# Expert stage of a fused attention and mixture-of-experts kernel: routing work moved between layers, weight pieces reordered

## The chip, the cores and the metric

The kernel runs on 1 core of one Trainium2 chip. The metric is the device time of one execution in microseconds (us). TensorE is called PE in the profile, VectorE is DVE, ScalarE is ACT, GpSimd is POOL, SyncE is SP (here it only starts DMAs). Each engine works through its own queue in order and meets the others at semaphores.

## What is computed

Three steps in a row. A recurrent attention (4 batches, 8 heads, 768 steps, width 40) gives 3072 rows of 320 numbers. A mixture of 8 experts then takes these rows, where each expert must get exactly 384 of them:

```python
logits = x @ w_gate
order = np.argsort(-logits.flatten())
for idx in order:                       # best (row, expert) pairs first
    tok, e = idx // E, idx % E
    if assigned[tok] >= 0 or counts[e] >= cap: continue
    assigned[tok] = e; counts[e] += 1
for e in range(E):
    h = np.maximum(x[assigned == e] @ w1[e], 0.0)
    out[assigned == e] = h @ w2[e]
```

The last step is one more network on every row, `g = elu(x @ w_in); y = g @ w_out`, of width 2048.

## The kernel before

**Stages.** The attention runs to about 206 us of the span and is not touched. `experts` then handles one expert after the other, in the order in which they fill up. For expert k it does a first layer pair (`up`, `down`: 320 to 1024 to 320) and, on the same 384 rows, the last network (`up2`, `down2`: 320 to 2048 to 320, called the second layer here). The hidden width is cut in slices of 128: 8 slices u in the first layer (`NF`), 16 slices f in the second (`NF2`). Every product is made of high and low parts: 8 matmuls of 384 columns for a slice of `up`, `down` or `up2`, 9 matmuls of 320 columns for a slice of `down2`.

**A second-layer slice on four engines.** PE makes `up2(f)` into one of three PSUM banks (`ring`). ACT makes negation, tanh and exp of it (`elu` on ACT), DVE combines them in two instructions (L1274, L1277), ACT rounds the result to its high part `gl_hi` (L1405), POOL subtracts to get the low part `gl_lo` (L1024), and PE multiplies both in `down2(f)`, three slices behind (`LAG`). `up2(f)` for f of 3 or more waits until DVE has finished slice f - 3, whose bank it writes into: `pe.wait_ge(g_ok, k * NF2 + f - 2)`.

**Routing.** The rows of expert k + 1 are found while expert k is computed. DVE and PE alternate in 7 rounds (`ROUNDS`): DVE compares all scores with up to 31 thresholds (`round_compare`, L1112), PE counts the takers with 24 small matmuls (`count_takers`, L1463), DVE tests (`round_test`), PE counts the thresholds passed with one matmul (`count_thresholds`, L1469), DVE moves the base (`round_move`). Then follow `choose_counts`, `totals` (PE), `choose_expert` (which also releases the weight fetch of that expert on SP), `prefix` (PE), `choose_ties`, `prefix` again, `choose_leave`, `choose_spots` (24 DVE instructions, L1233, that fill a one-hot table), `list_tokens` (24 matmuls, L1484) and `choose_tokens`, which gives the row numbers. POOL's `gather` fetches the rows with three indirect DMAs (L1003) and `columns` transposes them (PE L1495, ACT, DVE).

**Where it stands before.** Rounds 1 to 7 for the expert after next run in the second layer of expert k, one in every two slices; the rest of that routing in the first layer of expert k + 1. `choose_spots` stands in two halves at slices 6 and 7 of the first layer, its table shares memory with the buffers of the second layer (`unit`). Expert 0 has no expert ahead of it: its routing runs alone, and so do five rounds of expert 1.

**Weights.** SP fetches pieces into two staging buffers, ACT rounds the high part (`split_hi`), POOL subtracts for the low part (`split_lo`), and only then is the buffer free for the piece after next. The output weights `w_out` (8 pieces) come first, during the routing of expert 0. An expert's own 8 pieces (4 of `w1`, then 4 of `w2`) are worked on in the second layer of the expert before, one at every even slice.

## Time and profile before

| | us |
|---|---|
| median of 3 runs (lowest, highest) | 885.33 (883.17, 887.6) |
| the profiled execution | 887.74 |
| its span, first to last instruction | 886.0 |
| PE busy in the span | 790.1 |
| DVE, ACT, POOL busy | 527.8, 461.4, 421.1 |

The span is what the trace shows; 1.7 us lie around it. A busy PE is a PE with a matmul in its pipeline, so gaps count for more than the share. The span has three parts: attention to about 206 us, a stretch in which PE is mostly idle to about 264 us, and then eight experts, one about every 77 us.

### The profile page before, as it was taken

To read this page: it belongs to the slowest core of one execution; us is meant where nothing else is said; L and a number is where in the kernel's file an instruction comes from. 1 tells how busy PE (TensorE), PEld (TensorE's weight loads), DVE (VectorE), ACT (ScalarE), POOL (GpSimd) and SP (SyncE) were. 2 spreads that over 40 slices of the span, in tenths; PEclk is the share of its full clock that TensorE was granted. 3 is DMA by queue.
4 is the path that set the end of the run, shared out by engine and by line. 5 is a ranking of instruction groups with operands and counts; after the bars stand their busy time and mean duration, and the time that the engine had idled before them with its cause. 6 is when DMAs were issued, how large, how long until landed. Compare 5 with 4: busy or idle time off the path is not lost.

```text
span 886.0 us, 19502 instructions
## 1 busy us (share of the span) xinstructions
PE 790.1 (89%) x6470; PEld 734.4 (83%) x6470; DVE 527.8 (60%) x1535; ACT 461.4 (52%) x981; POOL 421.1 (48%) x467
## 2 busy tenths in 40 slices
PE   1999999994249999999999999999999999999994
PEld 1788888883139899989989989998999899899894
DVE  7475666666774864765476476547647655543441
ACT  1444444431231676387277538726763872784573
POOL 6444444443360475085257508525750852474133
PEclk9999999996557999999999999999999999999998
DMA  3978787842241120121212012121201211120000
GB/s 65 143 135 137 130 135 129 138 79 89 88 124 42 45 67 23 58 80 46 65 46 66 31 53 80 43 68 44 67 24 58 80 46 65 46 79 24 0 2 22
DMA packets 138521, 61.12 MB, mean 69 GB/s; under 512 B 104704, under 2 KB 136704, under 8 KB 138432
## 3 DMA queue, kind: packets, MB, share of 16 engines
q1 hardware_dynamic: 136128, 52.13, 27.1%
q0 software_dynamic: 2304, 7.87, 2.8%
q8 instruction: 48, 0.79, 0.4%
q14 instruction: 41, 0.34, 0.1%
HBM read 51.72 MB, written 8.26 MB: 68 GB/s over the span
## 4 chain that ended last, share of the span: by engine, by line
PE 54%; DVE 7%; POOL 5%; issue 4%; ACT 4%; DMA 1%; SPq 1%; ACTq 0%; POOLq 0%; DVEq 0%
PE bank L1503 6%; PE bank L1573 6%; PE bank L1504 5%; PE bank L1507 5%; PE bank L1574 5%; PE bank L1575 5%; PE bank L1463 3%; PE bank L1511 3%; PE bank L1509 3%; PE bank L1547 3%; PE bank L1549 3%; PE bank L1548 3%; DVE cmp L1112 2%; POOL gl_lo L1024 1%; PE bank L1532 1%
## 5 line engine op out<-in xcount | busy, mean ns | idle before, releaser
L1024 POOL TENSOR_TENSOR gl_lo<-unit,gl_hi 128x384 fp32r<-128x384 f32 x128 | 133.8, 1045 | 128.0 <-ACT gl_hi L1405 127.4
L1573 PE MATMUL bank<-Wo_hi,gl_hi 128*128 128x320 f32 x384 | 123.7, 322 | 5.0 <-POOL gl_lo L1024 5.0
L1574 PE MATMUL bank<-Wo_lo,gl_hi 128*128 128x320 f32 x384 | 118.7, 309 | 0.0
L1575 PE MATMUL bank<-Wo_hi,gl_lo 128*128 128x320 f32 x384 | 118.7, 309 | 0.0
L1274 DVE SCALAR_TENSOR_TENSOR unit<-bank,unit 128x384 f32<-128x384 f32 x104 | 57.8, 556 | 94.2 <-ACT bank L1398 93.9
L1373 ACT ACTIVATE hid_hi<-bank 128x384 fp32r<-128x384 f32 x64 | 31.4, 491 | 133.7 <-PE bank L1511 133.7
L1003 POOL DMA_INDIRECT xg<-x_rows,idx x24 | 23.7, 989 | 157.9 <-PE bank L1511 90.4
L1503 PE MATMUL bank<-x_hi,Wi_hi 128*128 128x384 f32 x256 | 92.3, 360 | 2.0 <-DVE unit L1277 0.9
L1390 ACT ACTIVATE unit<-bank 128x384 f32<-128x384 f32 x128 | 62.0, 484 | 51.3 <-PE bank L1511 50.2
L1504 PE MATMUL bank<-x_hi,Wi_lo 128*128 128x384 f32 x256 | 86.2, 337 | 0.0
L1573 PEld LDWEIGHTS bank<-Wo_hi,gl_hi 128*128 128x128 f32 x384 | 72.2, 188 | 6.8 <-POOL gl_lo L1024 6.7
L1277 DVE TENSOR_TENSOR unit<-unit,bank 128x384 f32<-128x384 f32 x128 | 70.9, 554 | 4.4
L1574 PEld LDWEIGHTS bank<-Wo_lo,gl_hi 128*128 128x128 f32 x384 | 72.2, 188 | 0.0
L1575 PEld LDWEIGHTS bank<-Wo_hi,gl_lo 128*128 128x128 f32 x384 | 72.1, 188 | 0.0
L1393 ACT ACTIVATE unit<-unit 128x384 f32<-128x384 f32 x128 | 67.3, 525 | 4.4
L1463 PEld LDWEIGHTS bank<-pick,cmp 128*128 128x128 bf16 x1344 | 38.4, 99 | 36.0 <-DVE cmp L1112 24.7
L1405 ACT CAST gl_hi<-unit 128x384 fp32r<-128x384 f32 x128 | 63.8, 499 | 6.3 <-DVE unit L1277 6.2
L1463 PE MATMUL bank<-pick,cmp 128*128 128x8 bf16 x1344 | 43.3, 167 | 25.6 <-DVE cmp L1112 25.3
L1257 DVE SCALAR_TENSOR_TENSOR hid_lo<-bank,hid_hi 128x384 fp32r<-128x384 f32 x64 | 35.4, 554 | 51.4 <-ACT hid_hi L1373 50.8
L1507 PE MATMUL bank<-x_lo,Wi_hi 128*128 128x384 f32 x256 | 65.9, 339 | 0.0
L316 POOL TENSOR_SCALAR_AFFINE_SELECT W<-W 128x512 f32<-128x512 f32 x48 | 35.4, 761 | 61.2 <-ACT W L490 61.2
L442 DVE TENSOR_TENSOR PW<-bank,W 128x512 f32<-128x512 f32 x48 | 30.9, 686 | 50.2 <-PE bank L551 45.6
(244 smaller groups left out, 2122.8 us busy)
## 6 DMA issues: line engine op xcount, KB each, us to landing
stage<-in_moe_w_dram SPq DMA_DIRECT2D x32, 320.0 KB, 2.9
stage<-in_moe_w_dram SPq DMA_DIRECT2D x32, 256.0 KB, 2.6
stage<-in_moe_w_dram SPq DMA_DIRECT2D x96, 64.0 KB, 2.4
q_in<-in_q_dram SPq DMA_DIRECT2D x24, 160.0 KB, 3.2
k_in<-in_k_dram SPq DMA_DIRECT2D x24, 160.0 KB, 3.9
o_in<-in_o_gate_dram SPq DMA_DIRECT2D x24, 160.0 KB, 4.1
v_in<-in_v_dram SPq DMA_DIRECT2D x24, 160.0 KB, 4.1
x_rows<-xt SPq DMA_DIRECT2D x24, 160.0 KB, 1.9
```

The costliest lines, as they stand in the source:

```text
L1024: nc.gpsimd.tensor_tensor(gl_lo[:, b, :], ex[:, b, :], gl_hi[:, b, :].bitcast(F32), ALU.subtract).then_inc(gl_ok, 1)
L1277: nc.vector.tensor_tensor(ex[:, b, :], ex[:, b, :], ring[(NF + f) % 3][:, 0:CAP], ALU.max).then_inc(g_ok, 1)
L1390: nc.scalar.activation(ex[:, b, :], ring[(NF + f) % 3][:, 0:CAP], ACT.Relu, scale=-1.0).then_inc(neg_ok, 1)
L1393: nc.scalar.activation(th[:, f % 2, :], ex[:, b, :], ACT.Tanh, scale=-0.5).then_inc(th_ok, 1)
L1405: nc.scalar.copy(gl_hi[:, b, :], ex[:, b, :]).then_inc(gl_hi_ok, 1)
L1463: ins = nc.tensor.matmul(pR[:, 0:E], cmp_w[:, g * NT:g * NT + P], pick[:, g, :], start=(g == 0), stop=(g == G - 1))
L1503: nc.tensor.matmul(to, w_hi[:, c, cols], x_hi[m][:, c, :], start=(c == 0), stop=False)
L1504: nc.tensor.matmul(to, w_lo[:, c, cols], x_hi[m][:, c, :], start=False, stop=False)
L1507: nc.tensor.matmul(to, w_hi[:, c, cols], x_lo[m][:, c, :], start=False, stop=False)
L1573: nc.tensor.matmul(acc[j][:, 0:DM], gl_hi[:, f % RG, t_], Wo_hi[:, f, :], start=(f == 0), stop=False)
L1574: nc.tensor.matmul(acc[j][:, 0:DM], gl_hi[:, f % RG, t_], Wo_lo[:, f, :], start=False, stop=False)
L1575: ins = nc.tensor.matmul(acc[j][:, 0:DM], gl_lo[:, f % RG, t_], Wo_hi[:, f, :], start=False, stop=(f == NF2 - 1))
```

## The change

- Of the 7 rounds for the next expert only rounds 1 and 2 stay in the second layer of the expert before (slices 11 to 15). Rounds 3 to 7 stand at slices u = 2 to 6 of the first layer, `choose_counts` to `choose_ties` at its end.
- `choose_leave` and both halves of `choose_spots` stand on DVE between the two layers, ahead of slice 0 of the second; `spot` has a buffer of its own. `list_tokens` stands on PE behind `up2(3)`, `choose_tokens` on DVE ahead of slice 3, `gather` on POOL behind slice 1. `TURN`, the slice of the first transposes, goes from 12 to 9.
- The high part `gl_hi` of even slices is made by DVE instead of ACT.
- Pieces of an expert come in the order of `PIECES`; five of them are worked on in the second layer of the expert before (slices 0, 4, 6, 8, 10), three in the expert's own first layer (u = 2, 3, 4).
- `w_out` is fetched behind the pieces of expert 0: three pieces are worked on in the first layer of expert 0 (u = 5, 6, 7), five in its second (slices 0, 1, 3, 4, 5). Ahead of expert 0 POOL has the gather first, then five pieces.
- Ahead of the first matmul only rounds 1 and 2 of expert 1 remain, and the three transposes stand together.

```diff
-    spot = unit[:, 0:G * P // 2].bitcast(FP16).rearrange("p (g c) -> p g c", g=G)
+    spot = sb("spot", [P, G, P], FP16)
...
+    PIECES = ((True, 0), (True, 1), (False, 0), (True, 2), (False, 1), (True, 3), (False, 2), (False, 3))
+    EARLY = 5
...
+    def in_up(k, u):
+        own = [(None, EARLY + u - 2)] if u - 2 < PER - EARLY else []
+        late = [(u - 5, None)] if isinstance(k, int) and k == 0 and u >= 5 else []
+        return own + late
+    def in_up2(k, f, after):
+        if isinstance(k, int) and k == 0:
+            outs, at = (0, 1, 3, 4, 5), (7, 9, 11, 13, 15)
+        else:
+            outs, at = (), (0, 4, 6, 8, 10)
...
-    TURN = NF2 - NJ - 1
+    TURN = 9
...
@@ gpsimd
-                gather(k + 1, 1 - s)
             for f in range(NF2):
                 elu_lo(k, f)
-                if f % 2 == 0 and after:
-                    expert_rest(k + 1, f // 2)
+                for i, at in in_up2(k, f, after):
+                    w_out_rest(i) if at is None else expert_rest(k + 1, at)
+                if f == 1 and after:
+                    gather(k + 1, 1 - s)
...
@@ vector
             for u in range(2, NF):
+                q = u + 1
+                if after and q <= ROUNDS:
+                    round_compare(c, q)
+                elif after:
+                    choose_counts(c)
+                hidden(k, u - 1)
+                if after and q <= ROUNDS:
+                    round_test(c, q)
+                    round_move(c, q)
+            if after:
+                choose_expert(c)
+            hidden(k, NF - 1)
+            if after:
+                choose_ties(c)
             between_layers(k)
             if after:
-                choose_tokens(c, 1 - s, n + s)
+                choose_leave(c)
+                for part in range(SPOTS):
+                    choose_spots(c, part)
             for f in range(NF2):
+                if f == 3 and after:
+                    choose_tokens(c, 1 - s, n + s)
...
@@ tensor
                 up(k, u)
+                if after and q <= ROUNDS:
+                    count_takers(c, q)
...
                 down(k, u - 2)
+                if after and q <= ROUNDS:
+                    count_thresholds(c, q)
...
                 if f < NF2:
                     up2(k, f)
+                if f == 3 and after:
+                    list_tokens(c)
```

How the rows stand in the queues. First DVE, from the end of the first layer of expert 0 to its first second-layer slice; `x_lo1` is the input of the second layer, `hid_lo` a slice of the first. Before:

```order
L1233 TENSOR_SCALAR unit<-slots,row 128x128 x12
L1257 SCALAR_TENSOR_TENSOR hid_lo<-bank3,hid_hi 128x384
L1233 TENSOR_SCALAR unit<-slots,row 128x128 x12
L1257 SCALAR_TENSOR_TENSOR hid_lo<-bank4,hid_hi 128x384
...
L1268 TENSOR_TENSOR x_lo1<-unit,x_hi1 64x384
...
L1274 SCALAR_TENSOR_TENSOR unit<-bank6,unit 128x384
L1277 TENSOR_TENSOR unit<-unit,bank5 128x384
```

And after the change:

```order
L1301 TENSOR_TENSOR x_lo1<-unit,x_hi1 64x384
L1233 SCALAR_TENSOR_TENSOR L<-taken,L 128x192
...
L1256 SCALAR_TENSOR_TENSOR L<-sel,L 128x192
L1266 TENSOR_SCALAR spot<-slots,row 128x128 x24
L1307 SCALAR_TENSOR_TENSOR unit<-bank6,unit 128x384
L1310 TENSOR_TENSOR unit<-unit,bank5 128x384
L1314 CAST gl_hi<-unit 128x384
L1307 SCALAR_TENSOR_TENSOR unit<-bank6,unit 128x384
```

The 24 instructions of `choose_spots`, and the 10 of `choose_leave` ahead of them, moved from among the slices of the first layer to a place between `x_lo1` and the first slice of the second layer.

Then POOL, from the start of the second layer of expert 1. Before:

```order
L1003 DMA xg<-x_rows,idx0 128x320 x3
L1024 TENSOR_TENSOR gl_lo<-unit,gl_hi 128x384
L764 TENSOR_TENSOR W1_lo<-stage0,W1_hi 128x2x256
L767 TENSOR_TENSOR W1_hi<-stage0,W1_hi 128x256
L1024 TENSOR_TENSOR gl_lo<-unit,gl_hi 128x384 x2
```

And after the change:

```order
L1056 TENSOR_TENSOR gl_lo<-unit,gl_hi 128x384
L764 TENSOR_TENSOR W1_lo<-stage0,W1_hi 128x2x256
L767 TENSOR_TENSOR W1_hi<-stage0,W1_hi 128x256
L1056 TENSOR_TENSOR gl_lo<-unit,gl_hi 128x384
L1028 DMA xg<-x_rows,idx0 128x320 x3
L1056 TENSOR_TENSOR gl_lo<-unit,gl_hi 128x384 x3
```

The gather moved from ahead of `gl_lo` of slice 0 to between those of slices 1 and 2.

Last PE, from the transposes of expert 0's rows to its first products. Before:

```order
L1495 MATMUL bank6<-ident,xg 64x128
L1463 MATMUL bank7<-pick,cmp 128x8 x24
L1469 MATMUL bank7<-feas,first31 128x1
L1495 MATMUL bank6<-ident,xg 128x128 x2
L1495 MATMUL bank6<-ident,xg 64x128
L1463 MATMUL bank7<-pick,cmp 128x8 x24
L1469 MATMUL bank7<-feas,first15 128x1
L1503 MATMUL bank3<-x_hi0,W1_hi 128x384
```

And after the change:

```order
L1537 MATMUL bank6<-ident,xg 64x128
L1537 MATMUL bank6<-ident,xg 128x128 x2
L1537 MATMUL bank6<-ident,xg 64x128
L1505 MATMUL bank7<-pick,cmp 128x8 x24
L1545 MATMUL bank3<-x_hi0,W1_hi 128x384
```

The counts that stood between and behind the transposes are gone from here, but for one.

## Rows read from the trace of the kernel before

**Rows 1.** page, part 1: busy us (share of span) xinstructions, by engine
```profile
PE 790.1 (89%) x6470; PEld 734.4 (83%) x6470; DVE 527.8 (60%) x1535; ACT 461.4 (52%) x981; POOL 421.1 (48%) x467
```

**Rows 2.** windows: busy us per engine in each, PE clock, DMA share, GB/s
```profile
206.00:232.00 26.00, 8.38 (x181) 7.00 (x181) 14.83 (x43) 5.80 (x8) 13.79 (x11) 0.50 0.35 103
...
272.00:277.00 5.00, 4.56 (x17) 4.42 (x16) 2.47 (x12) 0.49 (x1) 0.00 (x0) 0.50 0.00 2
...
277.00:282.00 5.00, 5.00 (x33) 4.84 (x32) 1.83 (x11) 0.49 (x1) 0.00 (x0) 0.99 0.00 0
...
380.00:460.00 80.00, 78.88 (x633) 74.07 (x634) 49.83 (x156) 49.85 (x109) 42.38 (x42) 1.00 0.18 54
```

**Rows 3.** timeline, first routing: start us, us, engine, line, out<-in, [idle before]
```profile
213.59 1.53 POOL L770 TENSOR_TENSOR Wo_lo<-stage,Wo_hi 128x640 fp32r<-128x640 f32 x1
...
213.73 2.19 DVE L1112 SCALAR_TENSOR_TENSOR cmp<-hi,base,ramps 128x744 bf16<-128x744 f32 x1
...
238.00 6.66 DVE L1233 TENSOR_SCALAR unit<-slots,row 128x128 f16<-128x128 f16 x24
...
240.73 1.30 POOL L764 TENSOR_TENSOR W_lo<-stage,W_hi 128x512 fp32r<-128x512 f32 x1 [8.55 <-ACT W_hi L755]
```

**Rows 4.** line L1112, one form: ns min/median/max, first to last start
```profile
L1112 DVE SCALAR_TENSOR_TENSOR cmp<-hi,base,ramps x16: 1024/1039/2235, 213.7 to 700.1; 128x744 bf16<-128x744 f32 x16
```

**Rows 5.** timeline, from routing of expert 1 to second layer of expert 0
```profile
246.02 0.34 DVE L1071 TENSOR_REDUCE best<-L 128x24 f32<-128x192 f32 x1
...
254.36 0.88 PE L1495 MATMUL bank<-ident,xg 128*128 128x128 f32 x3
...
261.58 0.87 PE L1495 MATMUL bank<-ident,xg 128*128 128x128 f32 x3
...
264.46 0.66 PE L1503 MATMUL bank<-x_hi,W_hi 128*128 128x384 f32 x1
...
295.72 0.42 PE L1503 MATMUL bank<-x_hi,Wi_hi 128*128 128x384 f32 x1
```

**Rows 6.** timeline, PE, threshold count 3 and taker count 4, expert 0
```profile
221.17 0.19 PE L1469 MATMUL bank<-feas,first 128*128 128x1 bf16 x1 [0.43 <-DVE feas L1122]
...
223.07 0.81 PE L1463 MATMUL bank<-pick,cmp 128*128 128x8 bf16 x24 [1.71 <-DVE cmp L1112]
```

**Rows 7.** timeline, DVE, around the start of a steady second layer
```profile
439.27 0.21 DVE L1206 TENSOR_TENSOR_SCAN incl<-bank,zeros 128x24 f32<-128x24 f32 x1 [2.02 <-PE bank L1479]
...
441.15 0.56 DVE L1257 SCALAR_TENSOR_TENSOR hid_lo<-bank,hid_hi 128x384 fp32r<-128x384 f32 x1
...
444.04 2.03 DVE L1233 TENSOR_SCALAR unit<-slots,row 128x128 f16<-128x128 f16 x12
...
450.05 0.55 DVE L1268 TENSOR_TENSOR x_lo<-unit,x_hi 64x384 fp32r<-64x384 f32 x1 [0.51 <-ACT x_hi L1383]
...
452.91 0.56 DVE L1274 SCALAR_TENSOR_TENSOR unit<-bank,unit 128x384 f32<-128x384 f32 x1 [0.52 <-ACT bank L1398]
...
453.50 0.56 DVE L1277 TENSOR_TENSOR unit<-unit,bank 128x384 f32<-128x384 f32 x1
```

**Rows 8.** timeline, PE, the same second layer
```profile
454.11 0.45 PE L1503 MATMUL bank<-x_hi,Wi_hi 128*128 128x384 f32 x1 [0.24 <-DVE unit L1277]
...
455.62 0.76 PE L1463 MATMUL bank<-pick,cmp 128*128 128x8 bf16 x24
...
463.24 0.39 PE L1573 MATMUL bank<-Wo_hi,gl_hi 128*128 128x320 f32 x1
```

**Rows 9.** timeline, POOL, the same second layer
```profile
454.65 1.07 POOL L1003 DMA_INDIRECT xg<-x_rows,idx  x1 [0.31 <-issue]
...
456.76 1.31 POOL L764 TENSOR_TENSOR W_lo<-stage,W_hi 128x512 fp32r<-128x512 f32 x1
...
458.01 0.76 POOL L767 TENSOR_TENSOR W_hi<-stage,W_hi 128x256 fp32r<-128x256 f32 x1
```

**Rows 10.** waits of PE after 277 us: total us, times, longest us
```profile
PE bank L1463 <- DVE cmp L1112: 2.1, 3, 1.0
```


## What I predict, and why

> **What bounds the kernel now.** I read the busy shares first, then the windows by stage, then the timeline of three places. PE is busy for 790 of 886 us [rows 1]: the kernel is bound by PE wherever PE can work. The windows show where it can't. From 206 to about 264 us it has a matmul in flight for a small part of the time (8.4 of the first 26 us) and runs at a granted clock of 0.5, the level of 1.2 GHz; in the middle of the expert stage it is busy for 78.9 of 80 us at 1.00, 2.4 GHz [rows 2]. So there are two prices. A microsecond cut from the serial stretch before the first expert is a microsecond gained. In the steady part nothing can be gained beyond some 1 us of waiting for each expert (78.9 of 80), and any new wait of PE is paid in full, seven times, since seven of the eight experts carry the routing of a next one.
>
> **The start: a gain of about 9 us.** Ahead of expert 0 the change takes all work from POOL and ACT that does not belong to the routing. What is it worth? DVE's comparison with `base` takes 2.19 us beside POOL's subtraction, which began 0.14 us before it [rows 3]; the median of this form is 1.04 us [rows 4]. Two such comparisons run in the first routing: 2 x 1.15 = 2.3 us. The 24 instructions of `choose_spots` took 6.66 us there, beside POOL's splits of `w1` [rows 3], and 2.03 us for 12 in the steady part, where POOL is idle [rows 7]: 6.66 - 4.06 = 2.6 us. With 0.3 us for the last comparison the routing of expert 0 ends 5.2 us earlier, and that of expert 1 begins at 240.8 instead of 246.0 [rows 5].
>
> From there to the first product before: 264.46 - 246.02 = 18.4 us [rows 5]. After: the first transposes have one round less ahead of them. A round is a comparison of 1.04, a count of 0.81 and three small steps, about 3 us in all (0.19 + 1.71 us from threshold count to taker count are the shorter part of one [rows 6]). So they start 254.36 - 246.02 - 3.0 = 5.3 us behind the routing's begin, at 246.1. The row of the last transposes is followed by the first product 2.9 us later [rows 5]; without counts between, all three sets should keep this pitch (before they took 3.6): 246.1 + 3 x 2.9 = 254.8. That is 9.7 us earlier. The weights are ready: POOL does its gather from about 242 to 245.5 and needs 1.31 + 0.76 us for a `w1` piece [rows 9].
>
> From the first product to the second layer of expert 0 it took 295.72 - 264.46 = 31.3 us. Five rounds are added in there (count and restart about 0.9 each, 4.4 in all, and some 1.3 of waits, below); two rounds with PE waiting through most of them (about 1.3 each), the 24 matmuls of `list_tokens` (0.6) and part of the stretch at 1.2 GHz go (about 2). I take +0.5, so the second layer of expert 0 starts **9.2 us earlier**. Bounds of this term: 6 if weight pieces, which now come three to the first layer, hold `up` or `down` once; 12 if the clock rises early.
>
> **The second layer: a new wait of about 4 us, then one of 2.** This is the term that decides. Before, DVE finishes `x_lo` at 450.05 + 0.55 = 450.6, has 2 us of small routing work, and takes slice 0 at 452.91, when ACT's exp is ready [rows 7]. PE has by then done three slices into the three banks of `ring`; its fourth starts at 454.11, just behind DVE's second instruction, after an idle 0.24 us [rows 7, 8]. So DVE's slice 0 is already what PE meets first.
>
> The change puts `choose_leave` and all of `choose_spots` ahead of that slice, in the same queue. `choose_leave`: 441.15 - 439.27 = 1.9 us for the part behind the prefix and 0.3 for two instructions ahead of it; `choose_spots`: 2 x 2.0 us [rows 7]. Together 6.2 us, from 450.6 to 456.8. Slice 0 then ends at 456.8 + 1.15 = 457.95 instead of 454.06, and `up2(3)` starts at **457.9, not 454.1: 3.8 us later**, behind 4 us of an idle PE. Nothing can fill them: PE's next instruction is this one, and its data are in no other engine's hands.
>
> Then POOL. Before, the gather is issued while nothing else wants POOL; its last issue starts at 454.65 and `gl_lo` of slice 0 follows. Now it stands behind slice 1, and behind a piece of `w1`. DVE's new cast of `gl_hi` has no row; it reads and writes 384 columns in SBUF. Its bounds are 0.2 (12 one-source instructions of 128 columns take 2.03, 0.17 each) and 0.56, what the two-operand instructions of 384 columns take [rows 7]; I take 0.35, nearer to the one-source rows. Then: 457.95 + 0.35 = 458.3; `gl_lo(0)` to 459.35 (1.0 us, the distance of slice 0's to the next row of POOL); the piece, 1.31 + 0.76 with a little overlap, to 461.4 [rows 9]; `gl_lo(1)` to 462.4; the gather, three issues of about 1.27, to 466.4; `gl_lo(2)` to 467.5. PE needs it for `down2(2)`. Counted from 457.9, it has `up2(3)`, `up2(4)`, `up2(5)` at 1.4 (454.11 to 455.62 is 1.5 with a restart [rows 8]), `list_tokens` 0.6 and two `down2` of 1.4, and gets there at 465.5. So it waits 2.1 us more, to about 467.7. Before, `down2(2)` started at 463.24 [rows 8]. PE is 4.45 us later, and has one count (0.8 with its restart) less behind it: 5.25 us of new waiting. The waits of the comparisons that leave this layer were 2.1 us in all after 277 us [rows 10], 0.35 for each expert. **Net 4.9 us for each of 7 experts, 34.3 us.** For expert 0 POOL has a second piece of `w_out` ahead of the gather (1.57 instead of nothing, less 0.5 for the smaller first one): +1.1.
>
> DVE's cast takes from ACT 0.5 us every second slice. ACT was no bound (49.9 of 80 us [rows 2]), so this gives nothing; DVE (49.8) has room for it.
>
> The row of 2.19 us bears on that cast: DVE stood still until POOL was through [rows 3]. The Trainium skill (SBUF — State Buffer, section Terms) has the rule: VectorE and GpSimd share one pair of ports, exclusively for a whole instruction, and the loser is blocked. By it the cast of slice 2 would wait out the piece of `w1` and hold POOL for itself, 0.4 us more before `gl_lo(2)`, 2.8 us over seven experts; without it nothing. The sum is made with half of that, inside the 467.7.
>
> **The first layer.** Rounds 3 to 7 now stand between `up` and `down`. PE's work for them is the same as in the second layer. Their chain runs from the threshold count through DVE's move and comparison to the next taker count, and has only one `up` of 1.4 us to hide in. For round 4, with its two more instructions, it is 223.07 - 221.17 = 1.9 us [rows 6]: a wait of 0.5. Rounds 5 to 7 have half as many thresholds and fit, but two of them meet a weight piece on POOL and can be held by up to its 1.31 us [rows 9]; I take 0.3 each. The first taker count covers 0.2 us that `down(0)` waited before. Net 0.9 us, for six experts 5.4 (expert 0's are in the term above). Bounds: 0 and 3 us for each expert.
>
> **The sum**, against the profiled execution: 887.7 - 9.2 + 34.3 + 1.1 + 5.4 = 919.3. The median of the runs is 2.4 us below that execution: **917 us**, 3.6% slower.
>
> **Rivals.**
> (1) The clock falls in the new wait of 4 us. Where PE was idle for stretches of a microsecond and more, it ran at 0.50, and came back to 1.00 only after it had worked without a gap from about 272.5 to 277 [rows 2]. In the 5 us before it did 17 matmuls, in the 5 us behind 33: such a stretch loses 2.5 us. A part is absorbed by the wait for POOL behind it; with a second fall there I take 2 us net for an expert: 917 + 14 = 931, up to 938 with 3 us. Against it: idle of half a microsecond never lowered it in the steady part [rows 2], and for 4 us there is no row. The Trainium skill (TensorE: Matmul & The Clock Gate, section Why this matters for your kernels) warns that idle gaps between bursts of matmuls bring the lower clock back; by it the time would be this rival's 931, by the rows it is open.
> (2) POOL keeps up: the first piece or the gather costs PE no second wait. Then 2.2 us less for each expert, 917 - 15 = 902. For it: POOL's times are rough; against it: three issues in a row stand in its queue.
> (3) Faster than before: the start decides. This needs less than 9.2 / 7 = 1.3 us of new waiting for each expert, so DVE would have to be through with `choose_leave` and `choose_spots` in about 3.5 us, not 6.2, because exp(0) came later or the 24 instructions ran faster from their own buffer. With no such wait the time is 885.3 - 9.2 + 5.4 - 2.5 = 879. Against it: the fastest rows for 12 of them are 2.03 us.
>
> **How the numbers follow.** My forecast with its own range (908 to 926) has 0.52, rival 1 0.20, rival 2 0.14, rival 3 0.08, something between before and 900 that I don't see 0.06. The range reaches to rivals 1 and 2 and leaves out rival 3 and the ends: 899 to 938. Beyond 0.5% (4.4 us, about what a measurement of this kernel can tell from no change): faster 0.08, within 0.03, slower 0.89.
>
> **What would show it.** In the changed profile: the first product at about 255 us; the comparisons of the first routing at 1.0 us; 24 `spot` instructions in 4 us right before DVE's slice 0, and PE idle about 4 us before the fourth slice of each second layer, put down to DVE; then about 2 us put down to POOL's `gl_lo`; a second-layer period of 81 to 83 us for each expert instead of 77. I am wrong if PE's longest waits there are under 1.5 us, or if the clock row shows levels under 1.00 in the steady part.

## The result, and the profile after

The changed kernel takes **942.2 us** (939.6 to 942.6, four runs) where the kernel before takes 886.5 on the same chip (883.2 to 892.0, four runs): a ratio of **1.062**, 95% interval 1.056 to 1.067. The forecast was 917 us with a range of 899 to 938. The direction, the start and the main wait came as forecast. The size didn't: 25 us of loss were missed, more than the range allowed.

The page of the changed kernel, part 1, as [rows 1]:

```profile
PE 806.9 (86%) x6470; PEld 745.6 (79%) x6470; DVE 593.1 (63%) x1599; ACT 436.1 (46%) x917; POOL 422.5 (45%) x467
```

PE has the same 6470 instructions, is busy 17 us longer for them (790.1 before) and idle 37 us longer (133 against 96 us). The longer work for the same matmuls goes with the lower clock: the mean granted clock is 0.941 over 940.1 us, where it was 0.955 over 886.0, so 55 us of full clock are missing instead of 40. The windows say where (us, then busy us of PE, PEld, DVE, ACT, POOL, then PE clock, DMA share, GB/s): one of 80 us as in [rows 2], one inside the new wait, and one behind each of two waits.

```profile
380.00:460.00 80.00, 72.94 (x582) 68.02 (x581) 53.01 (x134) 43.18 (x92) 39.63 (x38) 0.96 0.18 53
...
386.50:390.30 3.80, 0.03 (x1) 0.00 (x0) 3.77 (x20) 1.16 (x4) 0.00 (x0) 1.00 0.00 0
...
391.40:394.60 3.20, 3.20 (x35) 2.96 (x34) 2.95 (x9) 2.34 (x5) 3.20 (x4) 0.56 0.00 0
447.00:449.80 2.80, 2.80 (x10) 2.49 (x10) 0.40 (x3) 0.00 (x0) 1.38 (x2) 0.50 0.41 117
```

In 80 us PE is busy for 72.9 where it was for 78.9. It is idle from 386.5 to 390.3 at full clock, works on, and about 1.4 us later the clock goes to 0.50, its level of 1.2 GHz. The same happens again behind a shorter wait at 446 us.

Waits of PE behind 277 us, as [rows 10] (total us, times, longest us). Before, the longest in the steady part were about 1 us.

```profile
PE bank L1545 <- DVE unit L1310: 27.0, 7, 3.9
PE bank L1505 <- DVE cmp L1145: 10.6, 6, 2.1
PE bank L1537 <- DVE unit L1307: 6.3, 6, 3.5
PE bank L1617 <- POOL gl_lo L1056: 4.9, 8, 2.1
```

The first line is the fourth slice of each second layer, the second the comparison of round 4 in the first layer (2.0 to 2.1 us in five experts, 0.4 in the sixth), the third the transposes of the next tokens, the fourth `down2`. Together they are 49 us; the loss is 56. Here is the first of them in the timeline (start us, us, engine, line, out<-in, idle before); it stands where [rows 7, 8] stood before:

```profile
382.69 0.55 DVE L1301 TENSOR_TENSOR x_lo<-unit,x_hi 64x384 fp32r<-64x384 f32 x1 [0.50 <-ACT x_hi L1422]
383.17 0.34 DVE L1233 SCALAR_TENSOR_TENSOR L<-taken,L 128x192 f32<-128x192 f32 x1
...
385.29 4.00 DVE L1266 TENSOR_SCALAR spot<-slots,row 128x128 f16<-128x128 f16 x24
389.19 0.55 DVE L1307 SCALAR_TENSOR_TENSOR unit<-bank,unit 128x384 f32<-128x384 f32 x1
389.78 0.55 DVE L1310 TENSOR_TENSOR unit<-unit,bank 128x384 f32<-128x384 f32 x1
390.37 0.36 DVE L1314 CAST gl_hi<-unit 128x384 fp32r<-128x384 f32 x1
...
390.39 0.44 PE L1545 MATMUL bank<-x_hi,Wi_hi 128*128 128x384 f32 x1 [3.85 <-DVE unit L1310]
```

`choose_leave` takes 2.1 us, the 24 spots 4.0, slice 0 1.1, and PE waits 3.85 us: the forecast was 6.2 us of DVE work and 3.8 to 4 us of wait.

To compare periods, the matmul of `totals` is the best mark, since it stands once in each expert's routing. First the kernel before, expert 1 and expert 6, then the changed kernel:

```profile
355.12 0.29 PE L1473 MATMUL bank<-at_top,ones 128*128 128x16 f32 x2
...
742.04 0.29 PE L1473 MATMUL bank<-at_top,ones 128*128 128x16 f32 x2
```

```profile
282.43 0.29 PE L1515 MATMUL bank<-at_top,ones 128*128 128x16 f32 x2
...
376.41 0.29 PE L1515 MATMUL bank<-at_top,ones 128*128 128x16 f32 x2
...
803.41 0.29 PE L1515 MATMUL bank<-at_top,ones 128*128 128x16 f32 x2
```

The steady period, from expert 1's mark to the last, divided by five, was (742.04 - 355.12) / 5 = 77.4 us and is (803.41 - 376.41) / 5 = **85.4**. Expert 0's own (282.43 to 376.41) is **94.0** and was 76.2. From the second layer of expert 0 to that of expert 1 it is 93.8 us (287.41 to 381.22), 17.6 more than before. So each of the periods behind expert 0's loses about 8 us, and expert 0's loses 17.6 alone.

### The profile page after: what moved, and what is told of

It reads as the page before. It is cut to its first block, busy times and chain, and to the rows that moved or that the text cites. A ratio compares the mean times of both kernels' runs of the same rounds, so it can differ in the third digit from the quotient of the medians.

```text
span 940.1 us, 19480 instructions
## 1 busy us (share of the span) xinstructions
PE 806.9 (86%) x6470; PEld 745.6 (79%) x6470; DVE 593.1 (63%) x1599; ACT 436.1 (46%) x917; POOL 422.5 (45%) x467
## 4 chain that ended last, share of the span: by engine, by line
PE 41%; DVE 19%; issue 7%; POOL 5%; ACT 4%; DMA 0%; DVEq 0%; ACTq 0%; POOLq 0%; SPq 0%
PE bank L1545 4%; PE bank L1546 4%; PE bank L1549 4%; DVE cmp L1145 4%; PE bank L1505 4%; PE bank L1617 4%; PE bank L1619 3%; PE bank L1618 3%; DVE unit L1307 3%; PE bank L1589 2%; PE bank L1591 2%; PE bank L1590 2%; DVE spot L1266 2%; POOL xg L1028 2%; PE bank L1553 2%
## 5 line engine op out<-in xcount | busy, mean ns | idle before, releaser
L1618 PE MATMUL bank<-Wo_lo,gl_hi 128*128 128x320 f32 x384 | 121.1, 315 | 0.0
L1619 PE MATMUL bank<-Wo_hi,gl_lo 128*128 128x320 f32 x384 | 121.0, 315 | 0.0
L1307 DVE SCALAR_TENSOR_TENSOR unit<-bank,unit 128x384 f32<-128x384 f32 x104 | 57.7, 555 | 75.2 <-ACT bank L1437 74.6
L1429 ACT ACTIVATE unit<-bank 128x384 f32<-128x384 f32 x128 | 62.4, 487 | 86.0 <-PE bank L1553 83.5
L1617 PEld LDWEIGHTS bank<-Wo_hi,gl_hi 128*128 128x128 f32 x384 | 75.0, 195 | 8.0 <-POOL gl_lo L1056 4.2
L1618 PEld LDWEIGHTS bank<-Wo_lo,gl_hi 128*128 128x128 f32 x384 | 74.8, 195 | 0.0
L1545 PEld LDWEIGHTS bank<-x_hi,Wi_hi 128*128 128x128 f32 x256 | 49.0, 191 | 32.2 <-DVE unit L1310 29.6
L1619 PEld LDWEIGHTS bank<-Wo_hi,gl_lo 128*128 128x128 f32 x384 | 74.3, 193 | 0.0
L1310 DVE TENSOR_TENSOR unit<-unit,bank 128x384 f32<-128x384 f32 x128 | 70.9, 554 | 4.4
L1437 ACT ACTIVATE bank<-unit 128x384 f32<-128x384 f32 x104 | 51.6, 496 | 29.0 <-DVE unit L1307 20.9
L772 POOL TENSOR_TENSOR W_split<-stage,W_split 128x512 fp32r<-128x512 f32 x32 | 46.2, 1444 | 33.3 <-ACT W_split L756 33.3
## 6 DMA issues: line engine op xcount, KB each, us to landing
stage<-in_moe_w_dram SPq DMA_DIRECT2D x32, 256.0 KB, 2.6
```

Of the source, the lines that this page charges most:

```text
L1307: nc.vector.scalar_tensor_tensor(out=ex[:, b, :], in0=exp_at(f), scalar=1.0, in1=th[:, f % 2, :], op0=ALU.add, op1=ALU.mult).then_inc(em_o ...
L1310: nc.vector.tensor_tensor(ex[:, b, :], ex[:, b, :], ring[(NF + f) % 3][:, 0:CAP], ALU.max).then_inc(g_ok, 1)
L1429: nc.scalar.activation(ex[:, b, :], ring[(NF + f) % 3][:, 0:CAP], ACT.Relu, scale=-1.0).then_inc(neg_ok, 1)
L1545: nc.tensor.matmul(to, w_hi[:, c, cols], x_hi[m][:, c, :], start=(c == 0), stop=False)
L1617: nc.tensor.matmul(acc[j][:, 0:DM], gl_hi[:, f % RG, t_], Wo_hi[:, f, :], start=(f == 0), stop=False)
L1618: nc.tensor.matmul(acc[j][:, 0:DM], gl_hi[:, f % RG, t_], Wo_lo[:, f, :], start=False, stop=False)
```

## The experiments

All times in this table are medians, the difference is to the kernel before on the same chip in the same set, and the two last columns are read from the traces by the mark above (steady period; expert 0's period). Kernel before: 77.4 and 76.2.

| run | us | minus before | ratio, 95% | steady | expert 0 |
|---|---|---|---|---|---|
| changed kernel | 942.2 | +55.7 | 1.056-1.067 | 85.4 | 94.0 |
| a1_spots_behind | 946.2 | +55.7 | 1.059-1.065 | 86.6 | 96.4 |
| a2_no_late_pieces | 942.8 | +52.3 | 1.057-1.062 | 85.3 | 96.7 |
| a3_pe_kept_busy | 949.4 | +58.9 | 1.064-1.070 | 86.6 | 96.2 |
| a4_w_out_first | 954.4 | +63.9 | 1.069-1.076 | 88.2 | 88.3 |
| b1_routing_back | 896.9 | +7.2 | 1.006-1.010 | 78.4 | 85.5 |
| b2_back_w_out_first | 893.8 | +4.1 | 1.003-1.008 | 78.4 | 77.8 |
| b3_spots_alone | 949.1 | +59.5 | 1.062-1.068 | 86.5 | 89.3 |
| b4_spots_busy | 950.7 | +61.0 | 1.066-1.072 | 86.4 | 86.2 |
| c1_back_no_late | 887.3 | -0.1 | 0.998-1.001 | 77.6 | 77.5 |
| c2_wait4 | 911.0 | +23.6 | 1.023-1.029 | 80.9 | 80.0 |
| c3_wait4_busy | 902.3 | +14.9 | 1.015-1.020 | 79.9 | 79.3 |
| c4_wait2 | 891.2 | +3.8 | 1.002-1.006 | 77.6 | 76.8 |
| d1_no_spots | 926.1 | +37.7 | 1.040-1.046 | 82.7 | 91.9 |
| d2_no_spots_no_late | 921.7 | +33.3 | 1.035-1.042 | 81.7 | 94.6 |
| d3_spread_no_late | 937.1 | +48.8 | 1.051-1.057 | 84.4 | 98.2 |
| d4_late_by_two | 928.3 | +40.0 | 1.040-1.047 | 83.5 | 93.1 |
| e1_casts_back | 945.4 | +56.1 | 1.059-1.066 | 86.0 | 96.2 |
| e2_two_edits | 935.0 | +45.8 | 1.048-1.055 | 84.8 | 84.4 |

### First set: take one suspect at a time out of the changed kernel

**a1_spots_behind**: the spots stand behind the first slices.

```
             if after:
                 choose_leave(c)
-                for part in range(SPOTS):
-                    choose_spots(c, part)
             for f in range(NF2):
+                if f in (2, 3) and after:
+                    choose_spots(c, (2, 3).index(f))
# list_tokens, choose_tokens and gather from f = 1, 3 to f = 5; TURN 9 -> 11
```

> The changed kernel with the two halves of choose_spots moved behind slices 1 and 2 of the second layer (choose_leave stays ahead of slice 0), list_tokens and choose_tokens at slice 5, the gather behind slice 5, transposes at slice 11. Theory A: the wait of 3.9 us before up2(3), 27.0 us in seven experts of the changed kernel's trace, comes from these 24 instructions standing ahead of slice 0 on DVE; then it shrinks to under 0.5 us, and with it goes the short stretch of low clock behind it (1 to 1.5 us an expert): 942 - 24 to - 36 = 906 to 918 us. Rival B: DVE or POOL are short of time in the second layer anyway and the wait only moves to a later slice: less than 12 us gained.

The wait at the fourth slice is gone and nothing is gained. The waits of PE in this run, behind 277 us:

```profile
PE bank L1505 <- DVE cmp L1145: 20.1, 11, 3.5
PE bank L1526 <- DVE spot L1266: 10.5, 7, 1.5
PE bank L1545 <- DVE unit L1310: 8.7, 11, 2.0
```

Of the 27 us, 19 came back as waits of 1 to 2 us at the spots and at slices behind (the second and third line), and the wait for round 4 grew from 2.1 to 3.5 us in five of six experts. The rival held. The next run asks what holds round 4.

**a2_no_late_pieces**: for experts 1 to 7 all eight pieces are split in the second layer.

```
-        own = [(None, EARLY + u - 2)] if u - 2 < PER - EARLY else []
+        own = [(None, EARLY + u - 2)] if isinstance(k, int) and k == 0 and u - 2 < PER - EARLY else []
...
-            outs, at = (), (0, 4, 6, 8, 10)
+            outs, at = (), (0, 2, 4, 6, 8, 10, 12, 14)
```

> The changed kernel with all 8 weight pieces of experts 1 to 7 worked on in the second layer of the expert before, none in the first layer (expert 0 keeps its three). Theory A: the wait of about 2.1 us before the taker count of round 4 (10.6 us for six experts) comes from DVE's comparison being held by POOL's scatter and weight piece; without pieces the comparison takes 0.9 to 1.5 us instead of 2.7, the wait is 0.5 to 1.0, and the low clock behind it goes: 7 to 15 us gained, 927 to 935 us. Rival B: the chain itself is too long for one up slice (round 4 has two more instructions) and POOL has no part in it: no gain, 940 to 945, or slower by what the three extra pieces cost in the second layer.

The comparison of round 4, in the changed kernel and in this one (ns min/median/max, first to last start):

```profile
L1145 DVE SCALAR_TENSOR_TENSOR cmp<-lo,ramps x6: 933/2764/2818, 357.7 to 784.8; 128x744 bf16<-128x744 f32 x6
```

```profile
L1145 DVE SCALAR_TENSOR_TENSOR cmp<-lo,ramps x6: 932/934/934, 360.5 to 787.0; 128x744 bf16<-128x744 f32 x6
```

This shows the cause of the second wait: a weight piece on POOL. But the time stayed (52.3 against 55.7 us), as the rival had it: the second layer, now with eight splits, took back what the first gave.

**a3_pe_kept_busy**: 23 matmuls without use ahead of the fourth slice and 11 ahead of round 4's count.

```
+                if f == 3 and after:
+                    keep_busy(23, acc[0], Wi_hi, x_hi[1])
                 if f < NF2:
                     up2(k, f)
```

> The changed kernel with extra matmuls whose results nobody uses: 23 of 320 columns (about 3.4 us at the full clock) ahead of up2(3), 11 (1.6 us) ahead of the taker count of round 4. They fill PE's idle time and leave every wait for DVE and POOL where it is. Theory A (the low clock is a term of its own): the granted clock stays at 1.00 through the steady part, and each expert is 1 to 2.5 us shorter: 942 - 7 to - 17 = 925 to 935 us. Rival B (the low clock costs nothing, since PE is ahead of DVE and POOL behind these waits anyway): 940 to 945 us.

The mean granted clock rose from 0.941 to 0.960, and the time with it: +58.9 us instead of +55.7, above both theory and rival. PE reached `down2` earlier and waited there for POOL, 1.5 to 1.6 us in each steady second layer. So at that place of the changed kernel the lower clock and the wait for POOL stand in for each other:

```profile
PE bank L1621 <- POOL gl_lo L1056: 13.2, 8, 3.4
```

**a4_w_out_first**: the output weights are fetched and split ahead of expert 0 again, as before (`w_out_piece(i)` is `PI + i`, and SP, POOL and ACT take these pieces first).

> The changed kernel with the output weights fetched and split ahead of expert 0 again, as in the kernel before. Theory A: the second layer of expert 0, 10 us longer than those of the others in the changed kernel's trace (93.8 us to the next one against 85.5), is held by w_out's pieces, for which ACT waits up to 4.0 us with its slices queued behind; without them it takes 85 to 87 us, a gain of 7 to 9, while the routing of expert 0 gets 3 to 6 us longer from POOL's splits beside DVE's comparisons: 936 to 942 us, first product at 258 to 262 us instead of 256. Rival B: expert 0 is slow for another reason (gather, transposes): 945 to 948 us.

Expert 0's period fell from 94.0 to 88.3, nearly as the theory wanted. But the time, 954 us, is above theory and rival: the steady periods rose to 88.2, with the wait for round 4 at 3.5 us in five of six experts (17.5 us in all). Behind expert 0 the code of this run is that of the changed kernel. So the same code ran at periods of 85.4 and of 88.2 us, and a difference of this size between two runs isn't by itself the price of the edit. The first set so far: each suspect is real, and none of them alone gives its time back. The schedule answers to each edit elsewhere, so the next sets go the other way and build on the kernel before.

### Second set: which half of the change costs the time

**b1_routing_back** has all of the change but the places of the routing; **b2_back_w_out_first** also takes the output weights first.

```
# DVE and PE: body and first routing as in the kernel before
-    TURN = 9
+    TURN = NF2 - NJ - 1
...
+                gather(k + 1, 1 - s)
             for f in range(NF2):
```

> The changed kernel with the routing of the next expert back in the places of the kernel before (rounds in the second layer, tie-breaking, places and spots in the first, gather at the layers' border); the order of the pieces, the output weights behind expert 0 and VectorE's cast of every second slice stay changed. Theory (where the routing stands costs the time, the rest of the change costs nothing in the steady part): period of the second layers 77 to 78 us again, no wait of 3.9 us; the start gains about 5 us (2.2 for two comparisons and 2.6 for the spots of the first routing), expert 0 gives about 5 us back for the output weights: 886 us, 882 to 890. Rival (the pieces in order of need and the cast cost something for each expert): every period 0.5 to 1 us above 77.2, 891 us or more.

> As the run with the routing back, and the output weights are taken ahead of expert 0 again, as before. Theory: expert 0's period is 77 to 80 us, but the start loses about 3 us of its gain: 884 us, 880 to 888, the best of all if the 5 us of expert 0 were theirs. Rival (the output weights ahead take away the whole gain of the start): 887 us, the same as before.

Steady periods of 78.4 us instead of 85.4: **seven of the eight microseconds are the routing's place**. The rival held for the last one, and b2 missed both of its expectations (893.8 us; 884 and 887). In both runs PE waits about 1 us for each expert's first prefix, since `choose_expert` on DVE stands beside a late piece on POOL (c1, without late pieces, has no such wait). These are the waits of PE in b1:

```profile
PE bank L1615 <- POOL gl_lo L1057: 7.0, 8, 1.0
PE bank L1518 <- DVE eqs L1199: 4.7, 5, 1.0
PE bank L1575 <- DVE hid_lo L1290: 4.2, 2, 3.6
```

The third line is expert 0: `down` waits 3.6 us, until 291.7, for the low part of a hidden slice. It stands on DVE behind 12 spots, and these take 4.76 us (2.03 in [rows 7]) beside two splits of output weights on POOL:

```profile
286.31 4.76 DVE L1266 TENSOR_SCALAR spot<-slots,row 128x128 f16<-128x128 f16 x12
290.99 0.55 DVE L1290 SCALAR_TENSOR_TENSOR hid_lo<-bank,hid_hi 128x384 fp32r<-128x384 f32 x1
...
287.30 3.23 POOL L770 TENSOR_TENSOR Wo_lo<-stage,Wo_hi 128x640 fp32r<-128x640 f32 x2 [2.19 <-ACT Wo_hi L756]
```

b1 and b2 differ by 85.5 - 77.8 = 7.7 us in that period, and b2 starts it 2.9 us later (277.0 against 274.1). Between these two runs, the output weights fetched late cost more than they bring.

**b3_spots_alone** moves leave, spots and list in the kernel before; **b4_spots_busy** adds 24 matmuls of 320 columns ahead of the list.

```
-                    elif u == 5:
-                        choose_leave(c)
-                    elif u - 6 in range(SPOTS):
-                        choose_spots(c, u - 6)
                 hidden(k, u)
...
             between_layers(k)
+            if after:
+                choose_leave(c)
+                for part in range(SPOTS):
+                    choose_spots(c, part)
             for f in range(NF2):
                 q, odd = f // 2, f % 2
+                if f == 1 and after:
+                    choose_tokens(c, 1 - s, n + s)
                 if after == 2:
-                    if f == 0:
+                    if f == 1:
+                        choose_start(c + 1)
                         choose_keys(c + 1)
-                    elif f == 1:
                         round_compare(c + 1, 1)
```

> The kernel before with one thing of the change: VectorE does the places and the spots of the next expert between the layers and ahead of slice 0, not in the first layer; with them move the list of tokens (ahead of PE's fourth slice), the gather (behind slice 1) and the first step of the routing after it. Rounds stay in the second layer, pieces and casts as before. Theory (the wait ahead of the fourth slice and the half clock behind it make up about half of what the change lost): PE idle 3.3 to 4 us there, seven times, then 3.4 us at 0.50: 4 to 5 us for each expert, 886 + 28 to 35 = 917 us, 912 to 924. Rival A (the wait alone counts, and is partly absorbed behind it): 886 + 7 x 3.0 = 907 us. Rival B (nothing new: the wait only changes place with others of that layer): under 895 us.

> As the run with the spots alone moved, and 24 further matmuls of 320 columns (no result used) ahead of the list of tokens, so that PE is busy for most of the wait: 24 x 0.133 = 3.2 us at 2.4 GHz. Theory (the half clock behind the wait is a price of its own, about 1.5 us for each): no stretch at 0.50 between the experts, 7 x 1.5 us = 10 us less than the run with the spots alone. Rival (what the clock gives back is lost to a wait that comes right behind, for POOL): the same time as that run within 3 us, with PE waiting for gl_lo over 1 us more for each expert.

b3 is far slower than all it was expected to be. b4 takes the time of its rival, but the wait that fills up is not the rival's for `gl_lo`: it is the one for the comparisons, 31.1 us in 10 waits. The timeline of PE in b3 shows what the edit had overlooked:

```profile
479.43 0.76 PE L1483 MATMUL bank<-ids_at,spot 128*128 128x6 f16 x24 [2.81 <-DVE spot L1234]
...
486.36 0.81 PE L1462 MATMUL bank<-pick,cmp 128*128 128x8 bf16 x24 [3.31 <-DVE cmp L1113]
```

The first wait is the one meant (2.8 us for the spots). The second is new: the rest of the routing, whose first count stands two slices behind, follows late on DVE. So b3 and b4 price two waits at once and don't settle the price of one. They show only that rounds in the second layer and spots at its head don't go together. The other half alone, rounds moved and spots left in the first layer, was not run.

**c1_back_no_late** is b2 with a2's edit.

> As the run with the routing back and the output weights first, and for the experts 1 to 7 all eight weight pieces are split in the second layer, as before. What is left of the change is the order of the pieces, five of expert 0's ahead of its first layer, the cast of every second slice on VectorE, the buffer of its own for the spots and VectorE's reach over the first routing. In the run with three pieces in the first layer PE waited 1.0 us for the first prefix of each expert (VectorE's choice of the expert stands beside GpSimd's splits there). Theory: that wait goes, the periods are 77.3 us as before, and the 1.9 us of the earlier start stay: 0.998 of the kernel before, 887 to 888 us where that has 889.5. Rival (the cast or the order of need costs something): periods stay at 78, 1.005 as in that run.

The period is 77.6 and the time that of the kernel before (0.9997). So the order of the pieces, the cast on DVE and the buffer of its own for the spots cost nothing in the steady part (0.2 us a period at most). In its trace `totals` of expert 1 stands 3.9 us earlier than before (275.0 against 278.9), and 1.3 us of that goes in expert 0's period; the time of the runs, with an interval of 0.15% to both sides, shows no gain.

### Third set: the price of one wait

Nothing is moved here. 24 (or 12) further instructions of the form of `choose_spots` stand on DVE ahead of slice 0; in c3 PE also gets 29 matmuls of 320 columns.

```
+                if f == 0 and after:
+                    for g in range(24):
+                        nc.vector.tensor_scalar(again[:, g, :], slots[:], row[:, g:g + 1], None, ALU.is_equal)
                 elu(k, f)
```

> The kernel before, nothing moved; 24 further instructions of the form of choose_spots (into a buffer that nobody reads) stand on VectorE right ahead of slice 0 of the second layer: 24 x 0.169 = 4.06 us, the whole of which PE must wait at its fourth slice. It prices this one wait. Theory (wait and half clock): 4.0 of wait and 1.5 for the stretch at 0.50 behind it, 5.5 us for each of 7 experts: 889.5 + 38 = 928 us. Rival A (the wait alone): 7 x 4.0 = 28, 917 us. Rival B (more than that, since VectorE comes late to the slices and the rounds behind it): over 7 us for each, 939 us or more.

> As the run with 24 further instructions on VectorE, and PE is kept busy for the time of the wait by 29 matmuls of 320 columns (no result used), 29 x 0.133 = 3.9 us. No stretch at 0.50 behind it. Theory (the clock is a price of its own): about 10 us less than that run. Rival (VectorE or GpSimd are by then the slower ones, so PE at full clock waits for them instead): the same time within 3 us, and new waits for gl_lo or for slices behind.

> As the run with 24 further instructions on VectorE, with 12 of them: a wait of 2.0 us instead of 4.0. Theory: a wait of 2 us doesn't lower the clock, so 7 x 2.0 = 14 us, 903 to 905 us, and the 24 instructions cost more than twice as much as the 12. Rival (the clock falls in 2 us too): 7 x 3.5 = 24 us, 914 us.

c2, then c3: windows inside the wait and behind it.

```profile
461.70:465.20 3.50, 0.55 (x4) 0.23 (x2) 3.47 (x21) 1.39 (x4) 1.99 (x2) 1.00 0.45 119
466.00:468.50 2.50, 2.50 (x9) 2.19 (x9) 2.28 (x5) 2.44 (x6) 2.17 (x2) 0.50 0.00 0
```

```profile
455.60:459.00 3.40, 3.40 (x24) 3.40 (x23) 3.40 (x23) 1.65 (x4) 1.91 (x2) 1.00 0.44 111
461.00:464.00 3.00, 3.00 (x41) 2.84 (x40) 2.15 (x6) 2.94 (x7) 3.00 (x4) 1.00 0.02 5
```

DVE does the same in both. In c2 PE waits (23.1 us in 7 waits, longest 3.5) and then works at clock 0.50; in c3 it goes on at 1.00. The counts of matmuls can't be compared (24 of the 41 are the small ones of a taker count), but one slice can: the fourth, `up2(3)`, up to the count behind it, takes 468.49 - 465.76 = 2.73 us in c2 and 461.90 - 460.49 = 1.41 us in c3.

```profile
465.76 0.69 PE L1507 MATMUL bank<-x_hi,Wi_hi 128*128 128x384 f32 x1 [3.51 <-DVE unit L1278]
...
468.49 0.83 PE L1467 MATMUL bank<-pick,cmp 128*128 128x8 bf16 x24
```

```profile
460.49 0.34 PE L1507 MATMUL bank<-x_hi,Wi_hi 128*128 128x384 f32 x1
...
461.90 0.76 PE L1467 MATMUL bank<-pick,cmp 128*128 128x8 bf16 x24
```

The prices, for each of 7 experts: 23.6 / 7 = **3.4 us** for the wait with its clock, 14.9 / 7 = **2.1 us** with PE kept busy. So 1.2 us of the 3.4 are the clock's by the medians, 1.0 by the steady periods (80.9 and 79.9), and the slice above has 1.3; the 3.9 us of matmuls in c3 may outlast the wait by 0.4, which would add to it. The 12 instructions cost 3.8 / 7 = 0.5 us for 1.4 us of wait, at a clock of 1.00 throughout the windows of the middle. The cost isn't proportional: PE's small waits behind are taken in first. Between 277 and 880 us the waits at the fourth slice are 9.6 us instead of 0.9, and those for `gl_lo` and for comparisons 2.0 instead of 7.1, so 5.1 of the 8.7 us are absorbed. The theory had the order right and the sizes too high (38, 28 and 14 us were expected where 23.6, 14.9 and 3.8 came).

### Fourth set: both waits of the changed kernel

**d1_no_spots**: for experts 2 to 7 DVE does 2 of the 24 spots and the token list stays that of expert 1. **d2_no_spots_no_late**: with a2's edit. **d3_spread_no_late**: a1's and a2's edits together. **d4_late_by_two**:

```
# d1, d2
-            for g in range(part * n, (part + 1) * n):
+            for g in range(first, first + (n if isinstance(k, int) and k < 2 else 1)):
# d4, experts 1 to 7
-        own = [(None, EARLY + u - 2)] if u - 2 < PER - EARLY else []
...
+        if not (isinstance(k, int) and k == 0):
+            own = [(None, EARLY + u - 4)] if 0 <= u - 4 < PER - EARLY else []
```

> The changed kernel, and for the experts 2 to 7 VectorE does 2 of the 24 instructions of choose_spots (the token list stays that of expert 1: this part of the computation is left out). So 3.7 us go ahead of slice 0 of six second layers, and nothing takes their place. Theory (the costs add up): no wait of 3.9 us and no stretch at 0.50 behind it, 4.0 us less for each of six experts (the block's excess over its nominal time falls from 5.5 to 1.5 us): 942 - 24 = 918 us, 912 to 922. Rival (the waits stand in for each other: a slower engine sets the period): 935 us or more, with new waits for gl_lo, columns or comparisons.

> As the run without the spots, and no weight piece of the experts 1 to 7 is split in their first layer. Theory (costs add up): the comparison of round 4 takes 0.93 us, its wait falls from 2.1 us to under 1, the stretch at 0.50 behind it goes too: 2.5 us for each of six experts less than the run without the spots, 903 us, 898 to 908. Rival (as the run without late pieces alone showed: no gain): the same as the run without the spots, within 4 us.

> The changed kernel with the spots behind the first slices and without late pieces, two edits that gained nothing one by one (946 and 943 us). Theory (each took away its wait and met the other's): the wait of round 4, 3.5 us with the spots behind the slices, goes with its stretch at 0.50, about 4 us for each of six experts: 920 to 925 us. Rival (with all eight pieces GpSimd has no room for the splits, the gather and gl_lo in one layer): 940 us or more and waits for gl_lo of over 2 us for each expert.

> The changed kernel with the three late pieces of the experts 1 to 7 split two steps later in the first layer (behind the hidden slices 4, 5 and 6, not 2, 3 and 4), so that none stands beside the comparison of round 4. Theory: that comparison takes 0.93 us, its wait falls to about 0.7 and its stretch at 0.50 goes, 2.5 us for each of six experts less: 942 - 15 = 927 us, 922 to 932. Rival A (the rounds 5 to 7 are held instead): their comparisons, 0.5 us now, take 1.5 or more, and the time stays within 4 us of 942. Rival B (PE waits for the last piece of w1 or w2): slower than 942.

d4 takes 928.3 us, the 927 of its theory. PE's waits there, behind 277 us: the line of round 4 falls from 10.6 us to 1.2, the others stay.

```profile
PE bank L1547 <- DVE unit L1312: 27.1, 7, 3.9
PE bank L1539 <- DVE unit L1309: 5.6, 6, 3.0
...
PE bank L1507 <- DVE cmp L1147: 1.2, 6, 0.2
```

The span of its trace is 12.5 us shorter (927.6 against 940.1). The steady period fell by 1.9 us, five times, and expert 0's by 0.9, with 1.1 us lost behind the last mark. The remaining 3.2 us are an earlier mark (`totals` at 279.2 against 282.4) for which the edit gives no reason: it lies between 278.9 and 280.6 in seven of the nine traces that have the changed kernel's first part, and by the start of expert 0's second layer the two traces are level again (287.6 and 287.4). What these 3 us are stays open. So 9 to 10 us are shown for the wait of round 4 with its clock, some 1.6 for each of six experts; the wait alone fell by 9.4.

d1 took 22 of the 24 spots ahead of slice 0 away and gave 18.0 us back (55.7 to 37.7), 3.0 for each of six experts, not the 4.0 of the theory. Its waits behind 370 us say why:

```profile
PE bank L1620 <- POOL gl_lo L1057: 17.4, 6, 3.0
PE bank L1508 <- DVE cmp L1146: 3.0, 5, 2.0
```

Without the wait for the spots, PE waits 2.9 us at `down2(2)` for `gl_lo(2)`, behind a split and three issues of the gather on POOL. That is **the second wait of the forecast**, in its place. Its length is not the forecast's: in d1 POOL itself waits ahead of the gather for the row numbers (`idx`), 10.0 us in six times, which the forecast's chain hasn't. The cleaner measure is a3, where the spots stay, PE keeps its clock and the gather doesn't wait for `idx`: 1.5 to 1.6 us for each, 2.1 forecast. In the changed kernel the wait isn't seen (4.9 us in all, 2.1 once, in expert 0); PE comes there later, at half clock. d2 takes 4.4 us less than d1, where 15 were expected (five waits for round 4 were down to 3.0 us in d1 already, as the fence shows). d3 is 6.9 and 3.5 us better than its two edits alone, not 20. All three theories fell in size: the costs add up in part only.

### Last two

**e1_casts_back**: all casts of `gl_hi` on ACT. **e2_two_edits**: d4 with a4's edit.

```
# e1
-                nc.vector.tensor_copy(gl_hi[:, b, :], ex[:, b, :]).then_inc(gl_hi_dve, 1)
...
-                if f > 0 and f % 2 == 0:
+                if f > 0:
                     elu_hi(k, f - 1)
```

> The changed kernel with all casts of gl_hi on ScalarE again, as before; nothing else is undone. In the changed kernel VectorE's cast takes 0.36 to 0.54 us beside little work of GpSimd, 1.27 once for each expert and 4.1 us once in expert 0, beside two gl_lo, a split and issues of the gather. Theory (the casts cost PE nothing in the steady part, as the run with the routing back showed, and something in expert 0): periods stay at 85.4 us, expert 0 gets 0 to 4 us back: 938 to 942 us. Rival (VectorE is late in all second layers since the spots, so that each cast of 0.5 us at their start is paid): 1 us or more for each expert, under 935 us.

> The run with the late pieces two steps later (928.3 us), and the output weights taken ahead of expert 0 as before. Taken alone, this second edit made the changed kernel slower, 954 against 943 us, although expert 0's own period fell by 5.5 us: its steady periods were 88.5 instead of 85.4, with 3.5 us of waiting for round 4 instead of 2.1. Theory (that was the wait of round 4 in its longer form, and has gone with the pieces moved): start 3 us later, expert 0's period 5 us shorter, steady periods 83.2 as in the run with the pieces moved: 926 us, 923 to 929. Rival (the output weights first make the steady part slower in another way): 932 us or more.

e1 is 1.0625 of the kernel before where the changed kernel is 1.0616: the cast on DVE is no cause, not in expert 0 either, and neither theory nor rival (both faster) came. e2 missed its theory: 935, not 926. Its period of expert 0 is 8.7 us shorter than d4's and its start 7.5 us later (286.7 against 279.2), so up to expert 1 the place of the output weights is a matter of one microsecond; and its steady periods are 84.8, not 83.5, with some 1 us of waiting for a round-4 comparison that itself takes 0.93 us as it should. Why PE has the wait there and not in d4, with the same code behind expert 0, is open. No run beats the kernel before; c1 equals it.

## Why the prediction was right or wrong, point by point

- **The start: right.** First product at 256.0 (forecast 254.8), the first routing's comparisons at 0.93 to 0.99 us and its 24 spots at 3.99, as forecast, second layer of expert 0 at 287.4 instead of 295.7: 8.3 us earlier, 9.2 forecast.
- **The wait ahead of the fourth slice: right in place, length and releaser** (3.85 to 3.9 us, seven times, DVE L1310).
- **POOL's wait behind it: there only at full clock.** The term of 2.1 us assumed PE at full clock on its way there. With PE kept busy (a3) it is 1.5 to 1.6 us on top of the first wait; in the changed kernel the half clock takes its place. So the step gave a fair sum by a wrong route. (Its addition is 0.2 us too long besides: three issues of 1.27 behind 462.4 end at 466.2, not 466.4.) Rival 1, a fall of the clock, is what happened, and the prediction's own sign of being wrong, a level under 1.00 in the steady part, is there. It was priced net of this wait, at 2 us for each expert, and even its 931 to 938 us fall short. By c2 and c3 the clock's share behind one such wait is 1.0 to 1.3 us. The Trainium skill (TensorE: Matmul & The Clock Gate, section Why this matters for your kernels) warned that idle gaps between bursts of matmuls bring the lower clock back. The trace agrees for the waits of 3.85 us: a stretch at 0.50 lies at each of them. It fell at four of the five waits of 2.0 to 2.1 us for round 4 too, and at none of 1.4 us in c4.
- **The first layer: the step that failed first.** Its term was 0.9 us for each expert, with 0.5 for round 4. The trace has 2.0 us of wait in five of six experts, with a stretch at 0.50 at four of them; d4 gives back some 1.6 us for each of six. I had let the pieces on POOL hold "rounds 5 to 7", where the first piece meets round 4, the longest one; and had counted as cost the time that the piece runs, not that the comparison waits for it and only then does its own work:

```profile
443.40 2.72 DVE L1145 SCALAR_TENSOR_TENSOR cmp<-lo,ramps 128x744 bf16<-128x744 f32 x1
...
443.02 0.97 POOL L1035 DMA_INDIRECT out_dram<-yo,idx  x1 [0.30 <-issue]
444.01 1.27 POOL L764 TENSOR_TENSOR W_lo<-stage,W_hi 128x512 fp32r<-128x512 f32 x1
445.24 1.47 POOL L767 TENSOR_TENSOR W_hi<-stage,W_hi 128x256 fp32r<-128x256 f32 x1
...
446.19 0.79 PE L1505 MATMUL bank<-pick,cmp 128*128 128x8 bf16 x24 [2.00 <-DVE cmp L1145]
```

- **Expert 0: the step that failed most for its size.** Its period was to grow by 6.9 us (4.9 and 0.9 as every expert, 1.1 for one piece more on POOL). It grew by 17.6. Of the five pieces of output weights in that layer the forecast counted the two ahead of the gather, and only their time on POOL. The other three were left out, and so were all casts: they stand on ACT between the slices, and ACT waits in place for their transfers, with `elu` behind it:

```profile
303.02 0.73 ACT L756 CAST Wo_hi<-stage 128x640 fp32r<-128x640 f32 x1 [1.73 <-DMA stage<-in_moe_w_out_dram]
...
313.45 0.73 ACT L756 CAST Wo_hi<-stage 128x640 fp32r<-128x640 f32 x1 [3.96 <-DMA stage<-in_moe_w_out_dram]
```

  PE's own waits there are 2.1 and 1.0 us for `gl_lo` and 3.5 at the transposes, beside the 3.9 that every expert has; in a4 only 0.6 at the transposes is left of the three. Counted from second layer to second layer, taking the output weights first again gives 5.5 us back in a4 (93.8 to 88.3), 3.1 between b1 and b2 (81.0 to 77.9), 5.1 between d4 and e2 (89.5 to 84.4). No run parts what ACT's waiting costs from what POOL's splits cost.
- **The transposes: a term that was missing.** PE waits 0.6 us for each expert (DVE L1307) at `columns`, whose place the change moved to slices 9 to 11.
- **The cast: right.** 0.53 us in the middle, 0.35 assumed, within its bounds, and no time (e1). The rule on shared ports that stood with it, of which the forecast took half of 2.8 us, shows in rows (below); the casts' own share of the time is nothing that e1 could find.
- **The sum.** From one second layer to the next, the periods behind expert 0's grew by 8.9, 8.3, 7.2, 6.6 and 9.0 us, and the last part by 4.8: 44.8 us, where 6 x 4.9 + 5 x 0.9 = 33.9 were forecast, 10.9 too few. In the mean of experts 1 to 5 the second layer (first `up2` to last `down2`) grew by 2.0 us and the stretch between two of them by 6.0. Five counts less `list_tokens` changed sides, 3.4 us at the prediction's own prices (5 x 0.8 - 0.6). By this estimate the waits with their clock grew by 5.4 us in the second layer, 4.9 forecast, and by 2.6 in the first, 0.9 forecast: most of the 10.9 lies in the first layer. Expert 0's period grew by 10.7 more than forecast, and the start gave 0.9 less. With the 2.4 us by which the profiled execution of before lay above its median, and that of after doesn't, that is 24.9 of the 25 us.

## What to carry to other kernels

An order written out by hand has slack in particular places only. Before moving work, list for each place which queue it enters and what is queued behind it, on every engine that the moved work touches, DMA waits among them: here, in expert 0 alone, weight pieces that moved among the slices, with ACT waiting in place for their transfers and POOL splitting them, cost 3 to 6 us. And price a new wait of the matrix engine by an insertion of dummy work into the old kernel (c2 to c4): it is a small, clean run, and it says how much is absorbed (here over half of a short wait) and what the clock adds (here about a third of the price of a wait of 3.3 us), which no row of the old trace can say.

## What the runs showed of the hardware that I had not expected

- A comparison that reads and writes SBUF alone, issued 0.6 us before a split on POOL, lasted until 0.84 us behind the split's end: 2.72 us instead of 0.93, and POOL's next instruction took 1.47 instead of 0.75, the median of its form. In d4 it began in the same way during the issue of a scatter, with no split behind it, and took 0.93. So the one that begins first by the profile isn't always the one that goes first. The Trainium skill (SBUF — State Buffer, section Terms) says that VectorE and GpSimd share ports, one holding them for a whole instruction; the rows agree with the holding and show besides that an instruction counted as begun can be the one that is held.
- The same in the large: a cast of 0.36 us lasted 4.1 us in expert 0, beside the last issue of the gather, two `gl_lo` and a split on POOL. It cost nothing that e1 could give back.

```profile
306.43 4.11 DVE L1314 CAST gl_hi<-unit 128x384 fp32r<-128x384 f32 x1
...
306.81 1.96 POOL L1056 TENSOR_TENSOR gl_lo<-unit,gl_hi 128x384 fp32r<-128x384 f32 x2
308.73 1.58 POOL L770 TENSOR_TENSOR Wo_lo<-stage,Wo_hi 128x640 fp32r<-128x640 f32 x1
```

- Where the clock falls against a wait varies: 1.4 us behind the end of the wait at 390.4, 0.2 us behind that at 446.2, and once inside it (0.50 from 729.7 on, where PE waits until 731.1). At one wait of 2.1 us, which ends at 702.7, it didn't fall. A look at the clock inside the first wait (1.00 from 386.5 to 390.3) would have missed its price.

```profile
729.70:731.70 2.00, 0.61 (x2) 0.61 (x3) 1.84 (x6) 1.12 (x3) 0.10 (x1) 0.50 0.00 0
702.00:706.00 4.00, 3.31 (x40) 3.16 (x41) 2.38 (x7) 0.00 (x0) 2.90 (x3) 1.00 0.31 80
```
